# Attention, two dense layers with gates: tokens in five tiles instead of four batches, fills of one PSUM bank

## Chip, cores, metric
The kernel runs on one core of a Trainium2 chip. The metric is the device time of one execution in microseconds (us); smaller is better. TensorE is called PE here, its weight loads PEld, VectorE DVE, ScalarE ACT, GpSimd POOL, and the queue of SyncE, which issues the DMAs, SPq.

## What is computed
Attention over 4 batches of 8 heads, 576 tokens and 64 features per head, in which scores more than tau below the row's maximum are dropped, and then two feed-forward layers over all 2304 tokens:

```python
scores = q @ k.T / 8                                   # (4, 8, 576, 576)
scores = where(scores >= max(scores) - tau, scores, -1e9)
p = exp(scores - max(scores)); p = p / (sum(p) + 1e-9)
x = (p @ v) as 2304 tokens x 512
h = x @ w_in                                           # 512 -> 2048
y = (h * tanh(softplus(h))) @ w_out                    # 2048 -> 512
g = y @ w_gate; z = (silu(g) * (y @ w_val)) @ w_out2   # 512 -> 1536 -> 512
```

All operands are fp32. Each is split into a high part (rounded to fp32r) and a low part (the rest), and a product is three matmuls (high by high, high by low, low by high), or two where one operand holds both parts in its 128 rows.

## The kernel before
**Feed-forward work.** A unit is four 128x128 blocks of weights. There are 68 units per tile of tokens (UNITS): 16 for w_in, 16 for w_out, 24 for the gate and value matrices in turn (gate, value, gate, ...), 12 for the last matrix. A tile is one batch, 576 tokens, and a unit runs it in two halves of 288 columns, each 12 matmuls (4 blocks by 3 products, L455 to L457). A half fills 288 columns of a bank of ps_m, which has three banks in turn: a fill waits until the fill three before it has been read (`emptied`). For w_in, ACT reads the bank with Mish (mish, L652), ACT rounds to g_hi (g_high, L656) and POOL makes g_lo (g_low, L863). For a gate, ACT does tanh (L666) and DVE a product (gate_product, L773), and only then is the bank free; for a value, DVE reads it (s_product, L779), ACT makes g_hi and POOL g_lo (L867).

**Weights.** In tile 0 the 68 units are loaded raw (256 KB, load), rounded on DVE (w_high, L762), their low part made on POOL (w_low, L858), and stored split (512 KB, store, L422); in the other three tiles they are read back split (reload, L431). The ring w_sp has 6 slots, w_raw 3.

**Attention.** A pair of heads has 576 x 2 query rows in 9 chunks of 128: one chunk holds the last 64 rows of each of the two heads, with the products of both heads. For each chunk: scores (8 matmuls of 288 columns, or 4 if the chunk has one head; L481, L482) into a pair of banks, rowmax (L709) on DVE, exp (L628) on ACT, mask and sum (L717) on DVE, thresh and eps on POOL, reciprocal on DVE, norm (L848) on POOL. Then per head 25 transposes (L508, L511) in 6 turns, each one a bank of ps_x, each read by ACT (p_high, L638) and DVE (p_low, L731, L737), and 18 matmuls of 288 columns with v (values, L524 to L526), shifted on ACT (head_shift, L647) and added on DVE (head_add, L747). Per head, q, k and v are loaded into single buffers (load_qkv, L404 to L413) and split: q_high and q_low (L605, L702), k_high and k_low (L611, L824), v_high and v_low (L619, L830). After a batch, x_high (L754, DVE) and x_low (L853, POOL) make the input of its tile.

**Order.** Attention of batch 0 runs alone, with scores in two pairs of banks (ps_s and two banks of ps_m). Attention of batch a+1 is then mixed into the feed-forward units of tile a, with scores in one pair of banks (a chunk waits for the mask of the one before) and three banks of ps_x. The last tile has no attention beside it. The order of all steps on every queue is fixed at build time by `Plan.order`, a list scheduler with a cost, a rank and lags for each step; it picks the step that can start first. A step that needs the exp table is not put inside the 16 Mish units of a tile. Each engine works through its list in that order, with semaphore waits.

Of the kernel before, what the change touches and what calls it, by code (L numbers as in the profile page):

```python
# [11 lines left out]
P = 128  # L12
# [5 lines left out]
KC = 5  # L18
DC, FC1, FC2 = DM // P, F1 // P, F2 // P
UW = 4  # L20
KEY0 = (0, 128, 256, 384, 448)
CHUNKS = 9
P_SLOTS = 10
TURNS = 6
X_USES = TURNS + 2

# [10 lines left out]
W_RING = 6  # L37
W_RAW = 3
LEAD = 5
# [14 lines left out]
def p_slot(pair, ci):  # L54
    return 8 + pair % 2 if ci == 0 else ci - 1


def x_before(k):


    alone = X_USES * HEADS
    if k < alone:
        return k - 4
    return k - 3 if k - 3 >= alone else alone - 4 + k % 3


def unit_steps(u):

    if u in (0, U_G):
        return (0, 0), (1, 0), (0, 1), (1, 1)  # L70
    return (0, 2), (1, 2)


def unit_end(G):
    m, u = divmod(G, UNITS)
    return ("unit", m, u) + unit_steps(u)[-1]


class Plan:
# [12 lines left out]
    def attention(self, a):  # L92
        add = self.add
        alone = a == 0
        near = 0.15 if alone else 0.5
        for h in range(HEADS):
            H = HEADS * a + h
            J, odd = divmod(H, 2)
            q_used = ("scores", CHUNKS * (J - 1) + (8 if odd else 4))
            add("SP", 1.6, 2, ("load_qkv", H), (("q_low", H - 1), 0.1), (("k_low", H - 1), 0.1), (("v_low", H - 1), 0.1))  # L100
            add("ACT", 0.78, 5, ("q_high", H), (("load_qkv", H), 2.4), (q_used, 0.3))
            add("DVE", 0.9, 4, ("q_low", H), (("q_high", H), 0.2))
            add("ACT", 0.68, 5, ("k_high", H), (("load_qkv", H), 2.6), (q_used, 0.3))
            add("POOL", 1.75, 2, ("k_low", H), (("k_high", H), 0.2))
            add("ACT", 0.65, 6, ("v_high", H), (("load_qkv", H), 2.8), (("values", H - 2, 1), 0.3))
            add("POOL", 1.46, 4, ("v_low", H), (("v_high", H), 0.2))
        for j in range(PAIRS):
            J = PAIRS * a + j
            for ci in range(CHUNKS):
                C = CHUNKS * J + ci  # L110
                odd = ci > 4
                back = 2 if alone else 1
                kept = ("tpose", 2 * J - 3, 0) if ci == 0 else ("tpose", 2 * J - 2 + odd, TURNS - 1)
                add("PE", 1.06 if ci == 0 else 0.53, 1, ("scores", C), (("q_low", 2 * J + (ci == 0)), near),
                    (("k_low", 2 * J + (ci == 0)), near), (("mask", C - back), near))
                add("DVE", 0.75, 5, ("rowmax", C), (("scores", C), 0.3))
                add("POOL", 0.12, 0, ("thresh", C), (("rowmax", C), 0.15))
                add("ACT", 0.78, 3, ("exp", C), (("rowmax", C), 0.15), (kept, 0.3), table="exp")
                add("DVE", 0.85, 2, ("mask", C), (("exp", C), 0.2), (("thresh", C), 0.15))
                add("POOL", 0.12, 0, ("eps", C), (("mask", C), 0.15))  # L120
                add("DVE", 0.08, 1, ("recip", C), (("eps", C), 0.15))
                add("POOL", 1.0, 1, ("norm", C), (("recip", C), 0.15))
        for h in range(HEADS):
            H = HEADS * a + h
            J, odd = divmod(H, 2)
            held = ("values", H - (2 if alone else 1), 1)
            for i in range(TURNS):
                ready = ("norm", CHUNKS * J + (0 if i == 0 else 8 if odd else 4))
                add("PE", 0.55, 0, ("tpose", H, i), (ready, near), (self.x_free(H, i), near))
                add("ACT", 0.6 if i else 0.45, 2, ("p_high", H, i), (("tpose", H, i), 0.3), (held, 0.3))  # L130
                add("DVE", 0.68 if i else 0.5, 3, ("p_low", H, i), (("p_high", H, i), 0.2))
            for half in range(2):
                add("PE", 1.32, 0, ("values", H, half), (("p_low", H, TURNS - 1), near), (("v_low", H), near),
                    (self.x_free(H, TURNS + half), near))
                add("ACT", 0.42, 2, ("head_shift", H, half), (("values", H, half), 0.3))
                add("DVE", 0.45, 3, ("head_add", H, half), (("head_shift", H, half), 0.2))
        for j in range(PAIRS):
            y_used = ("unit", a - 1, U_O - 1, 1, 2)
            add("DVE", 0.5, 6, ("x_high", a, j), (("head_add", HEADS * a + 2 * j + 1, 1), 0.15), (y_used, 0.3))
            add("POOL", 1.65, 3, ("x_low", a, j), (("x_high", a, j), 0.2))  # L140

    def x_free(self, H, i):
        H, i = divmod(x_before(X_USES * H + i), X_USES)
        return ("p_low", H, i) if i < TURNS else ("head_add", H, i - TURNS)

    def weights(self, m):
        for u in range(UNITS):
            G = UNITS * m + u
            free = unit_end(G - W_RING)
            if m == 0:  # L150
                self.add("SP", 0.4, 1, ("load", G), (("w_low", G - W_RAW), 0.1), (unit_end(G - LEAD - 3), 0.1))
                self.add("DVE", 0.6, 4, ("w_high", G), (("load", G), 2.8), (free, 0.3), (("store", G - W_RING), 4.0))
                self.add("POOL", 1.47, 2, ("w_low", G), (("w_high", G), 0.2))
                self.add("SP", 0.4, 3, ("store", G), (("w_low", G), 0.1))
            else:
                self.add("SP", 0.4, 0, ("reload", G), (free, 0.1), (("store", G - W_RING), 4.0))

    def moe(self, m):
        add = self.add
        for u in range(UNITS):  # L160
# [7 lines left out]
            elif U_Y <= u < U_G:  # L168
                after.append((("g_low", m, UW * part + UW - 1), 0.3))
            elif u == U_G:  # L170
                after.append((("y_low", m, DC - 2, 1), 0.3))
                late = [(("y_low", m, DC - 1, 1), 0.3)]
            elif u >= U_O:
                after.append((("s_low", m, UW * part + UW - 1), 0.3))
            for half, blocks in unit_steps(u):
                each = late if blocks == 1 else after
                if first and blocks != 1:
                    each = each + [(self.emptied(2 * (FILLS * m + n) + half - 3), 0.3)]
                add("PE", (1.19, 0.4, 1.58)[blocks], 2, ("unit", m, u, half, blocks), *each)
            for half in range(2):  # L180
                done = (("unit", m, u, half, unit_steps(u)[-1][1]), 0.3)
                if u < U_Y:
                    add("ACT", 0.42, 0, ("mish", m, u, half), done, table="mish")
                elif u < U_G:
                    if end:
                        add("ACT", 0.42, 0, ("y_high", m, n - N_Y, half), done)
                        add("DVE", 0.45, 0, ("y_low", m, n - N_Y, half), (("y_high", m, n - N_Y, half), 0.2))
                elif u < U_O:
                    f, value = divmod(n - N_G, 2)
                    if not value:  # L190
                        add("ACT", 0.42, 0, ("gate_tanh", m, f, half), done, table="exp")
                        add("DVE", 0.45, 0, ("gate_product", m, f, half), (("gate_tanh", m, f, half), 0.2))
                    else:
                        add("DVE", 0.45, 0, ("s_product", m, f, half), done, (("gate_product", m, f, half), 0.15))
                elif end:
                    add("DVE", 0.45, 0, ("out", m, n - N_O, half), done)
            if u < U_Y:
                add("ACT", 0.68, 4, ("g_high", m, u), (("mish", m, u, 1), 0.2))
                add("POOL", 1.65, 1, ("g_low", m, u), (("g_high", m, u), 0.2))
            elif U_G <= u < U_O and (n - N_G) % 2:  # L200
                add("ACT", 0.68, 4, ("s_high", m, f), (("s_product", m, f, 1), 0.2))
                add("POOL", 1.55, 1, ("s_low", m, f), (("s_high", m, f), 0.2))
            elif u >= U_O and end:
                add("SP", 0.4, 0, ("keep", m, n - N_O), (("out", m, n - N_O, 1), 0.1))

    def emptied(self, k):
        F, half = divmod(k, 2)
        m, n = divmod(F, FILLS)
        if n < N_Y:
            return "mish", m, n, half  # L210
        if n < N_G:
            return "y_low", m, n - N_Y, half
        if n < N_O:
            f, value = divmod(n - N_G, 2)
            return ("s_product" if value else "gate_product"), m, f, half
# [712 lines left out]
```

## Time and profile before

| | us |
|---|---|
| median of 3 runs | 1235.16 (1234.11 to 1236.33) |
| the profiled execution | 1235.01, of which the span from the first to the last instruction is 1233.2 |
| first matmul starts | 26.55 |
| first feed-forward matmul starts | 168.64 |
| last matmul ends | about 1229.8 |

| engine | busy us | share of the span |
|---|---|---|
| PE | 1150.4 | 93% |
| DVE | 578.4 | 47% |
| POOL | 530.3 | 43% |
| ACT | 476.1 | 39% |

Matmuls are pipelined: a matmul's duration in the trace (about 295 ns for 288 columns) overlaps the next ones. What it costs in a full stream is its pitch, the time from one start to the next.

### The profile page before, as it was taken

The page shows a single profiled execution, that of the slowest core. Times are in us where ns is not written, and L with a number is a line of the kernel's source. Part 1 is how long each engine was busy: PE and PEld are TensorE (multiplying, and loading weights), DVE is VectorE, ACT ScalarE, POOL GpSimd, SP SyncE. Part 2 cuts the span into 40 slices and gives each one's busy share as a digit, 9 for nine tenths or more (in the row PEclk, how much of TensorE's full clock was granted, in tenths as well). Part 3 has the DMA queues.
Part 4 walks back from the last instruction along what each step waited for, and adds up shares of the span by engine and source line. Part 5 has one row for each costly group of instructions (what it writes and reads, how often), then busy time and mean ns, then how long its engine had stood idle before and what let it go on. Part 6 is the DMA issues. An engine that isn't in the chain of part 4 may idle for free.

```text
span 1233.2 us, 21754 instructions
## 1 busy us (share of the span) xinstructions
PE 1150.4 (93%) x8544; PEld 1133.3 (92%) x8544; DVE 578.4 (47%) x1240; ACT 476.1 (39%) x873; POOL 530.3 (43%) x698
## 2 busy tenths in 40 slices
PE   1666689999999999999999998999999999999998
PEld 0656579999999999999999998999999999999998
DVE  2787741366777850255666653045666400002220
ACT  1554544343444344434554435433444204302210
POOL 4455548756677835332444524432443304201210
PEclk9977789999999999999999999999999999999999
DMA  7111127665656554454545455544433465445443
GB/s 243 41 35 44 50 81 256 233 205 195 211 190 218 188 182 171 143 158 135 158 130 162 130 170 154 180 142 140 145 128 120 142 202 174 163 163 171 164 162 107
DMA packets 83765, 190.69 MB, mean 155 GB/s; under 512 B 29904, under 2 KB 29904, under 8 KB 83664
## 3 DMA queue, kind: packets, MB, share of 16 engines
q1 hardware_dynamic: 83664, 189.31, 47.6%
q8 instruction: 68, 1.11, 0.4%
q14 instruction: 33, 0.27, 0.1%
HBM read 148.90 MB, written 40.37 MB: 153 GB/s over the span
## 4 chain that ended last, share of the span: by engine, by line
PE 87%; DVE 5%; POOL 2%; ACT 2%; issue 1%; DMA 1%; SPq 1%; DVEq 0%; ACTq 0%
PE ps_m L455 23%; PE ps_m L457 23%; PE ps_m L456 23%; PE ps_x L511 5%; PE ps_s L481 3%; PE ps_s L482 3%; PE ps_x L524 2%; PE ps_x L525 2%; DVE p_t L717 2%; DMA k_raw<-kt 1%; DVE nmax L709 1%; PE ps_x L508 1%; DVE p_lo_b L737 1%; DVE p_lo L737 1%; PE ps_x L526 1%
## 5 line engine op out<-in xcount | busy, mean ns | idle before, releaser
L455 PE MATMUL ps_m<-x_hi,w_sp 128*128 128x288 f32 x1280 | 380.4, 297 | 5.9 <-ACT g_raw L652 3.3
L457 PE MATMUL ps_m<-x_hi,w_sp 128*128 128x288 f32 x1280 | 378.5, 296 | 0.0
L456 PE MATMUL ps_m<-x_lo,w_sp 128*128 128x288 f32 x1280 | 378.0, 295 | 0.0
L455 PE MATMUL ps_m<-g_hi,w_sp 128*128 128x288 f32 x896 | 265.3, 296 | 0.0
L457 PE MATMUL ps_m<-g_hi,w_sp 128*128 128x288 f32 x896 | 264.2, 295 | 0.0
L456 PE MATMUL ps_m<-g_lo,w_sp 128*128 128x288 f32 x896 | 263.9, 295 | 0.0
L455 PEld LDWEIGHTS ps_m<-x_hi,w_sp 128*128 128x128 f32 x1280 | 241.2, 188 | 7.2 <-ACT g_raw L652 3.8
L456 PEld LDWEIGHTS ps_m<-x_lo,w_sp 128*128 128x128 f32 x1280 | 241.2, 188 | 0.0
L457 PEld LDWEIGHTS ps_m<-x_hi,w_sp 128*128 128x128 f32 x1280 | 241.1, 188 | 0.0
L455 PEld LDWEIGHTS ps_m<-g_hi,w_sp 128*128 128x128 f32 x896 | 168.2, 188 | 0.3
L456 PEld LDWEIGHTS ps_m<-g_lo,w_sp 128*128 128x128 f32 x896 | 168.1, 188 | 0.0
L457 PEld LDWEIGHTS ps_m<-g_hi,w_sp 128*128 128x128 f32 x896 | 168.1, 188 | 0.0
L717 DVE SCALAR_TENSOR_TENSOR p_t<-ps_s,thr,p_t 128x576 f32<-128x576 f32 x126 | 102.7, 815 | 132.3 <-ACT p_t L628 119.2
L628 ACT ACTIVATE p_t<-ps_s,nmax 128x576 f32<-128x576 f32 x126 | 93.2, 740 | 169.5 <-DVE nmax L709 168.5
L863 POOL TENSOR_TENSOR g_lo<-g_raw,g_hi 128x576 fp32r<-128x576 f32 x64 | 91.6, 1432 | 111.3 <-ACT g_hi L656 111.2
L848 POOL TENSOR_SCALAR p_t<-p_t,rcp 128x576 f32<-128x576 f32 x144 | 108.5, 754 | 49.5 <-DVE rcp L724 48.7
L709 DVE TENSOR_REDUCE nmax<-ps_s 128x1 f32<-128x576 f32 x126 | 95.2, 755 | 69.1 <-PE ps_s L482 67.1
L867 POOL TENSOR_TENSOR g_lo<-g_raw,g_hi 128x576 fp32r<-128x576 f32 x48 | 69.9, 1457 | 128.6 <-ACT g_hi L670 128.3
L481 PE MATMUL ps_s<-k_hi,q_sp 128*128 128x288 f32 x280 | 87.4, 327 | 39.2 <-POOL k_lo L824 26.6
L638 ACT ACTIVATE p_hi<-ps_x 128x512 fp32r<-128x512 f32 (+2 forms) x164 | 87.9, 570 | 49.2 <-PE ps_x L511 43.8
L858 POOL TENSOR_TENSOR w_sp<-w_raw,w_sp 128x512 fp32r<-128x512 f32 x68 | 89.2, 1312 | 37.3 <-DVE w_sp L762 37.0
L652 ACT ACTIVATE g_raw<-ps_m 128x288 f32<-128x288 f32 x128 | 51.9, 411 | 133.5 <-PE ps_m L457 133.3
(91 smaller groups left out, 1575.4 us busy)
## 6 DMA issues: line engine op xcount, KB each, us to landing
w_sp<-scratch SPq DMA_DIRECT2D x204, 512.0 KB, 3.3
scratch<-w_sp SPq DMA_DIRECT2D x68, 512.0 KB, 3.0
w_raw<-weights SPq DMA_DIRECT2D x68, 256.0 KB, 3.4
q_raw<-qt SPq DMA_DIRECT2D x64, 144.0 KB, 3.7
k_raw<-kt SPq DMA_DIRECT2D x64, 144.0 KB, 3.7
out_t<-o_sb SPq DMA_DIRECT2D x16, 288.0 KB, 4.1
v_raw<-v SPq DMA_DIRECT2D x32, 128.0 KB, 2.7
v_raw<-v SPq DMA_DIRECT2D x64, 16.0 KB, 2.4
```

Source lines behind the costliest of these rows:

```text
L455: nc.tensor.matmul(ps, w_h, x_h, start=first, stop=False)
L456: nc.tensor.matmul(ps, w_h, x_l, start=False, stop=False)
L457: return nc.tensor.matmul(ps, w_l, x_h, start=False, stop=last)
L481: nc.tensor.matmul(to, q, k_hi[:, e, cols], start=e == heads[0], stop=False)
L628: act.activation(halves(p_t[:, slot, :]), s_banks(C), ACT.Exp, bias=nmax[:, slot:slot + 1]).then_inc(e_ready, 1)
L638: act.activation(to, from_ps, ACT.Copy).then_inc(p_hi_ready, 1)
L709: dve.tensor_reduce(nmax[:, slot:slot + 1], s_banks(C), axis=AX.XY, op=ALU.max, negate=True).then_inc(max_ready, 1)
L717: dve.scalar_tensor_tensor(p, s_banks(C), thr[:, slot:slot + 1], p, ALU.is_ge, ALU.mult, accum_out=sums[:, slot:slot + 1]).then_inc(mask_d ...
L848: pool.tensor_scalar(p_t[:, slot, :], p_t[:, slot, :], rcp[:, slot:slot + 1], 1.0, ALU.mult, ALU.mult).then_inc(norm_done, 1)
L858: pool.tensor_tensor(w_sp[:, slot, 1, :], w_raw[:, u % W_RAW, :], w_sp[:, slot, 0, :].bitcast(F32), ALU.subtract).then_inc(w_ready, 1)
L863: pool.tensor_tensor(g_lo[:, f, :], g_raw[:, f, :], g_hi[:, f, :].bitcast(F32), ALU.subtract).then_inc(g_lo_ready, 1)
L867: pool.tensor_tensor(g_lo[:, f, :], g_raw[:, f, :], g_hi[:, f, :].bitcast(F32), ALU.subtract).then_inc(s_lo_ready, 1)
```

## The change
- **Tiles.** The 2304 tokens are cut into five tiles of 384, 448, 512, 512 and 448, across the batches (TILES). Where a tile has tokens of two batches, attention for it is made in two pieces (PIECES). There are eight pieces, of 384, 192, 256, 320, 192, 384, 128 and 448 queries; each runs all 8 heads, with q of its queries and the whole k and v of its batch. So k and v are loaded and split for 64 heads, before for 32. The 144 chunks stay 144; 16 of them are still shared by two heads, 4 each in the pieces of 192, 320, 192 and 448.
- **Fills.** A unit runs its whole tile in one fill: 12 matmuls of 384 to 512 columns in one bank. ps_m has two banks in turn (M_BANKS), ps_x has two in turn beside feed-forward work (X_BANKS); in attention alone ps_x uses the two banks of ps_m as well. ps_s has four banks: scores use two pairs everywhere.
- **Transposes and values.** A head's 25 transposes are now 5 for each of its chunks (a shared chunk is turned whole for each head), in 5 turns of one block of keys, or 3 turns of two, two and one where they fit. values makes 9 matmuls of the piece's width.
- **Loads.** Two slots each for q, k and v; one DMA for each (the host writes q and k twice, one copy under the other, and lays v out as it lies in the buffer); k and q of a head are issued ahead of v and, for heads 0 to 2, ahead of the first weights. tau is loaded by ACT's queue, and the exp table is loaded at the start.
- **Weights.** Units with even numbers are raw in tile 0 alone and stored there. Units with odd numbers are raw in tiles 0 and 1 and stored in tile 1 (kept_at). So 102 raw loads, 68 stores, 238 reloads. w_high moves from DVE to ACT; w_low is on DVE for every second one and on POOL for the others. w_sp has 7 slots, w_raw 4.
- **The plan.** New costs; within an engine a step of lower rank may be taken if it can start within 0.2 us of the first; chunks of attention are held back so that they spread over 80% of the tile before (PACE).

```diff
-W_RING = 6
-W_RAW = 3
+W_RING = 7
+W_RAW = 4
+X_BANKS, M_BANKS = 2, 2
+TILES = (384, 448, 512, 512, 448)
+PACE = 0.8
+PATIENCE = {"PE": 0.0, "ACT": 0.2, "DVE": 0.2, "POOL": 0.2, "SP": 0.0}
+def kept_at(u):
+    return u % 2
+def low_on_vector(r):
+    return r % 2 == 1
+def turns_of(H):
+    n = queries(H)
+    if n == P:
+        return (0, 1, 2, 3), (4,)
+    if n + n % P <= 2 * P:
+        return (0, 1), (2, 3), (4,)
+    return (0,), (1,), (2,), (3,), (4,)
...
 def moe(self, m):
+        N = TILES[m]
+        mm = 3 * (0.231 if N == 512 else N / 2400 + 0.015)
...
-                back = 2 if C < CHUNKS * PAIRS else 1
-                if C >= back:
-                    pe.wait_ge(mask_done, C - back + 1)
+                if C >= 2:
+                    pe.wait_ge(mask_done, C - 1)
...
-            def load_qkv(H):
-                if H > 0:
-                    sp.wait_ge(q_ready, H)
-                for r in range(2):
-                    sp.dma_start(q_raw[r * DH:(r + 1) * DH, :], qt[H]).then_inc(q_loaded, 16)
...
+            def load_qk(H):
+                if H >= 2:
+                    sp.wait_ge(k_ready, H - 1)
+                sp.dma_start(k_raw[:, slot, :], kt[head]).then_inc(k_loaded[slot], 16)
+                if H >= 2:
+                    sp.wait_ge(q_ready, H - 1)
+                sp.dma_start(q_raw[:, slot, 0:n], qt[head, :, q0:q0 + n]).then_inc(q_loaded[slot], 16)
...
-                if first and blocks != 1:
-                    emptied(2 * (FILLS * m + n) + half - 3)
+                if first and not k0:
+                    emptied(FILLS * m + n - M_BANKS)
...
-                cols = slice(half * HALF, (half + 1) * HALF)
-                for k in (range(UW - 1), range(UW - 1, UW), range(UW))[blocks]:
+                for k in range(k0, k1):
                     w_cols = slice(k * P, (k + 1) * P)
-                    last = product(m_bank(m, n, half), w_sp[:, slot, 0, w_cols], w_sp[:, slot, 1, w_cols],
-                                   r_hi[:, cols], r_lo[:, cols], first and k == 0, end and k == UW - 1)
+                    last = product(m_bank(m, n), w_sp[:, slot, 0, w_cols], w_sp[:, slot, 1, w_cols], *rhs[k],
+                                   first and k == 0, end and k == UW - 1)
```

## Rows read from the trace of the kernel before
**Rows 1.** Page, 40 equal slices: busy tenths of PE, granted clock.
```profile
PE   1666689999999999999999998999999999999998
PEclk9977789999999999999999999999999999999999
```
**Rows 2.** Stretches: us, busy us (instructions) of the engines, granted clock, DMA share, GB/s.
```profile
26.50:168.60 142.10, 93.12 (x512) 83.06 (x512) 104.77 (x229) 71.44 (x125) 71.39 (x130) 0.82 0.17 47
168.60:1229.80 1061.20, 1057.26 (x8032) 1050.24 (x8032) 466.09 (x998) 399.72 (x741) 446.56 (x554) 1.00 0.51 167
...
168.60:300.00 131.40, 131.36 (x977) 130.55 (x978) 59.23 (x125) 53.99 (x100) 89.18 (x97) 0.98 0.63 211
300.00:430.00 130.00, 129.89 (x998) 128.51 (x997) 101.26 (x214) 57.96 (x108) 97.90 (x116) 1.00 0.60 200
```
**Rows 3.** Waits of PE from 168 us to the end: us in total, times, longest.
```profile
PE ps_m L455 <- ACT g_raw L652: 3.3, 1, 3.3
PE ps_m L455 <- POOL x_lo L853: 2.6, 1, 2.6
```
**Rows 4.** Chain that ended last, 0 to 30 us: start, us, what.
```profile
11.46 4.03 POOL w_sp L858 x3
...
16.35 1.11 SPq L404
...
19.03 0.60 SPq L408
...
19.67 4.55 DMA k_raw<-kt
...
24.25 0.69 ACT k_hi L611
...
25.01 1.41 POOL k_lo L824
...
26.55 0.58 PE ps_s L481
```
**Rows 5.** DVE in order of time, last tile: start us, us, operation, idle time before.
```profile
1199.62 0.46 DVE L787 COPY o_sb<-ps_m 128x288 f32<-128x288 f32 x1 [7.48 <-PE ps_m L457]
...
1209.16 0.46 DVE L787 COPY o_sb<-ps_m 128x288 f32<-128x288 f32 x1 [7.48 <-PE ps_m L457]
```
**Rows 6.** PE in order of time around twelve transposes.
```profile
300.34 1.47 PE L511 MATMUL ps_x<-ident,p_t 128*128 128x128 f32 x12
301.57 0.38 PE L481 MATMUL ps_s<-k_hi,q_sp 128*128 128x288 f32 x1
301.79 0.29 PE L482 MATMUL ps_s<-k_lo,q_sp 128*128 128x288 f32 x1
```
**Rows 7.** Groups by line and shape: count, busy us, mean ns, idle before.
```profile
L717 DVE SCALAR_TENSOR_TENSOR p_t<-ps_s,thr,p_t 128x576 f32<-128x576 f32 x126 | 102.7, 815 | 132.3 <-ACT p_t L628 119.2 <-POOL thr L836 12.2
L709 DVE TENSOR_REDUCE nmax<-ps_s 128x1 f32<-128x576 f32 x126 | 95.2, 755 | 69.1 <-PE ps_s L482 67.1
L628 ACT ACTIVATE p_t<-ps_s,nmax 128x576 f32<-128x576 f32 x126 | 93.2, 740 | 169.5 <-DVE nmax L709 168.5
L863 POOL TENSOR_TENSOR g_lo<-g_raw,g_hi 128x576 fp32r<-128x576 f32 x64 | 91.6, 1432 | 111.3 <-ACT g_hi L656 111.2
L858 POOL TENSOR_TENSOR w_sp<-w_raw,w_sp 128x512 fp32r<-128x512 f32 x68 | 89.2, 1312 | 37.3 <-DVE w_sp L762 37.0
...
L737 DVE TENSOR_TENSOR p_lo<-ps_x,p_hi 128x512 fp32r<-128x512 f32 x108 | 70.2, 683 | 22.6 <-ACT p_hi L638 22.4
...
L638 ACT ACTIVATE p_hi<-ps_x 128x512 fp32r<-128x512 f32 x108 | 59.1, 599 | 42.8 <-PE ps_x L511 42.5
...
L652 ACT ACTIVATE g_raw<-ps_m 128x288 f32<-128x288 f32 x128 | 51.9, 411 | 133.5 <-PE ps_m L457 133.3
...
L779 DVE SCALAR_TENSOR_TENSOR g_raw<-g_top,ps_m 128x288 f32<-128x288 f32 x96 | 43.5, 454 | 50.0 <-PE ps_m L457 49.5
```
**Rows 8.** x_high (L754) alone: count, durations in ns min/median/max, first and last start.
```profile
L754 DVE CAST x_hi<-x_raw x16: 450/460/1689, 62.3 to 978.2; 128x576 fp32r<-128x576 f32 x16
```

More of the change, by code:

```diff
@@ L97, in attention @@
             H = HEADS * a + h
[L98 to L103, printed above, removed]
@@ L104, in attention @@
-            add("POOL", 1.75, 2, ("k_low", H), (("k_high", H), 0.2))
-            add("ACT", 0.65, 6, ("v_high", H), (("load_qkv", H), 2.8), (("values", H - 2, 1), 0.3))
-            add("POOL", 1.46, 4, ("v_low", H), (("v_high", H), 0.2))
+            q_used = ("scores", chunks_of(H - 2)[-1]) if H >= 2 else None
+            add("SP", 0.8, 2, ("load_qk", H), (("q_low", H - 2), 0.1), (("k_low", H - 2), 0.1))
+            add("SP", 0.4, 2, ("load_v", H), (("v_low", H - 2), 0.1))
+            add("ACT", 0.2 + 0.00084 * SEQ, 5, ("k_high", H), (("load_qk", H), 2.4), (q_used, 0.3))
@@ L107, in attention @@
+            add("POOL", 1.45, 2, ("k_low", H), (("k_high", H), 0.2))
+            add("ACT", 0.2 + 0.00096 * n, 5, ("q_high", H), (("load_qk", H), 2.6), (q_used, 0.3))
+            add("DVE", 0.2 + 0.0012 * n, 4, ("q_low", H), (("q_high", H), 0.2))
+            add("ACT", 0.46, 6, ("v_high", H), (("load_v", H), 2.5), (("values", H - 2), 0.3))
+            add("POOL", 0.88, 4, ("v_low", H), (("v_high", H), 0.2))
         for j in range(PAIRS):
             J = PAIRS * a + j
[L109 to L122, printed above, removed]
@@ new lines, in attention @@
+            for C in range(FIRST[J], FIRST[J + 1]):
+                _, e, i = CHUNK[C]
+                H = 2 * J + (1 if e < 0 else e)
+                kept = ("tpose", last_reader(C - P_SLOTS), len(turns_of(last_reader(C - P_SLOTS))) - 1) if C >= P_SLOTS else None
+                pace = None
+                if not alone:
+                    first = FIRST[PAIRS * (LAST_OF[tile - 1] + 1)]
+                    last = FIRST[PAIRS * (LAST_OF[tile] + 1)]
+                    pace = unit_end(UNITS * (tile - 1) + int(PACE * UNITS * (C - first) / (last - first)))
+                add("PE", 1.06 if e < 0 else 0.53, 1, ("scores", C), (("q_low", H), near), (("k_low", H), near),
+                    (("mask", C - 2), near), (pace, 0.0))
+                add("DVE", 0.76, 5, ("rowmax", C), (("scores", C), 0.3))
+                add("POOL", 0.28, 0, ("thresh", C), (("rowmax", C), 0.1))
+                add("ACT", 0.74, 3, ("exp", C), (("rowmax", C), 0.1), (kept, 0.3), table="exp")
+                add("DVE", 0.9, 2, ("mask", C), (("exp", C), 0.15), (("thresh", C), 0.1))
+                add("POOL", 0.2, 0, ("eps", C), (("mask", C), 0.1))
+                add("DVE", 0.1, 1, ("recip", C), (("eps", C), 0.1))
+                add("POOL", 0.76, 1, ("norm", C), (("recip", C), 0.1))
@@ L123, in attention @@
         for h in range(HEADS):
             H = HEADS * a + h
[L125 to L140, printed above, removed]
@@ new lines, in attention @@
+            add("PE", 9 * max(0.1, n / 2400 + 0.015), 0, ("values", H), (("p_low", H, len(turns) - 1), near), (("v_low", H), near),
+                (self.x_free(USE0[H] + len(turns)), near))
+            add("ACT", 0.17 + 0.00084 * n, 2, ("head_shift", H), (("values", H), 0.3))
+            add("DVE", 0.17 + 0.00101 * n, 3, ("head_add", H), (("head_shift", H), 0.2), (("x_low", tile - 1, h // 2), 0.1))
+        if a == LAST_OF[tile]:
+            width = TILES[tile]
+            for j in range(PAIRS):
+                y_used = unit_end(UNITS * (tile - 1) + U_O - 1) if tile else None
+                add("DVE", 0.1 + 0.001 * width, 6, ("x_high", tile, j), (("head_add", HEADS * a + 2 * j + 1), 0.15), (y_used, 0.3))
+                add("POOL", 0.1 + 0.00236 * width, 3, ("x_low", tile, j), (("x_high", tile, j), 0.2))
@@ L180, in moe @@
[L180 to L196, printed above, removed]
@@ L197, in moe @@
-            if u < U_Y:
[L198 to L204, printed above, removed]
@@ L886, in _ @@
                     x_low(*args)
-                elif step == "w_low":
+                elif step == "w_low" and not low_on_vector(RAW_AT[args[0]]):
                     w_low(*args)
```

689 lines of the change are left out of this document (378 added, 311 removed).

## Prediction
> **What bounds the kernel now.** I read the slices of the page first, then the stretches, PE's waits, the chain that ended last, and single rows for prices. The slices split the run in two [rows 1]: up to 168.6 us PE is idle or six tenths busy at a reduced clock, and from there it is full. From 168.6 to 1229.8 PE is busy 1057.3 of 1061.2 us [rows 2], and only two of its waits count there, 3.3 and 2.6 us [rows 3]. So there are two regimes. In the first, 168.6 us long, the work of batch 0 is a chain through DVE, ACT and POOL: from 26.5 us on DVE is busy 104.8 of 142.1 us, 74%, more than any other [rows 2]. In the second, the time is PE's number of matmuls times their pitch. After the last matmul 3.4 us remain. The sum is made against the span, 1233.2; the execution took 1235.0, 1.8 more, and the median of the runs is 1235.2, so 1.8 is added at the end.
>
> **Start: 26.5 becomes about 8.5.** The chain shows who sets the first matmul [rows 4]: POOL does three w_low (11.5 to 15.5), the weights' queue entries follow, then q and k of head 1 are issued at 16.4 and 19.0, k lands at 24.2, ACT and POOL split it (0.7 + 1.4), and PE starts. Head 1 is needed at once because the first chunk is shared by two heads, and its load waits since there is one buffer. After the change head 0's k is first in the queue, head 1 has its own slot, and the piece of 384 has no shared chunk. Sum: issue at 1, landing 4.6 later, 0.7 + 1.4, waits between: 7.7; some transfers now meet, so I take 8.5 (bounds 7.7 and 11).
>
> **Attention alone: 142.1 becomes about 100.5.** 24 chunks instead of 36. A 128-row chunk costs DVE 0.755 + 0.815 + 0.16 for its reciprocal = 1.73 [rows 7]. DVE's other prices follow from two rows: 288 columns 0.454 and 512 columns 0.683 give 0.16 us plus 1.02 ns a column [rows 7], 0.55 for 384. So before: 36 x 1.73 = 62; turns 8 heads x 4.07 = 33; adds 16 x 0.454 = 7; q_low and x_high about 7: 109. After: 24 x 1.73 = 41.5; turns 8 x 5 x 0.55 = 22; adds 8 x 0.55 = 4.4; q_low, x_high and three w_low, which DVE gets, about 8.5: 76.5. Ratio 0.70; with the idle share kept, 142.1 x 0.707 = 100.5. Bounds: all of DVE's idle time stays (76.5 + 37.3 = 113.8), or a third of it goes with the shorter pairs (90). First feed-forward matmul: 8.5 + 100.5 = 109 instead of 168.6: **-59.6** (bounds -70 and -44). Nothing hides this: PE can do nothing before it.
>
> **Feed-forward matmuls.** Between two reads of finished sums lie 72 matmuls: 1209.16 - 1199.62 = 9.54, a pitch of 132.5 ns for 288 columns [rows 5]. At 2.4 GHz the columns are 120.0 of it, 12.5 come on top. Before: 68 x 12 x 2 x 4 = 6528 matmuls, 865.0 us. After: 68 x 12 x 5 = 4080, the same 2304 x 816 columns, 783.4 us of columns. If 12.5 ns stays per matmul: 783.4 + 51.0 = 834.4. If the extra grows with the columns (20 ns for 461): 865.0. No row shows more than 288 columns, and at 12 transposes of 128 columns the pitch is 0.103 [rows 6], so the extra is no constant below 288; I take the middle, 849.7: **-15.3** (bounds -30.6 and 0). The planner's new costs, 15 to 18 ns extra, say the same. The Trainium skill ("TensorE: Matmul & The Clock Gate", Wait — 56ns, not 53.3ns?) gives back-to-back matmuls N/2.4 ns plus about 2.5 ns; that would be 122.5 at 288 columns, and this trace has 132.5, so the row decides; by the page the sum after would be 793.6.
>
> **Attention that moves beside the feed-forward work.** Before, 24 heads were there; each costs PE 5 units of scores (a unit: 4 matmuls, 0.53) = 2.65, transposes 25 x 0.10 + 3 switches x 0.09 (the matmul after a run of transposes starts 0.22 later instead of 0.13 [rows 6]) = 2.77, values 18 x 0.1325 = 2.39: 7.8, 187 in all. Check: 865 + 187 = 1052 of the 1061.2 measured [rows 2]; 9 are left for the waits and the slow first matmuls. After, all but the first piece is there: scores 120 chunks, 16 of them double, 136 x 0.53 = 72; transposes 136 chunk readings x 5 = 680 x 0.10 = 68, and about 130 switches x 0.09 = 12, since two banks allow runs of two turns; values 72 matmuls for each of seven pieces at 0.118, 0.128, 0.148, 0.118, 0.176, 0.109 and 0.203 (192, 256, 320, 192, 384, 128, 448 columns, between the pitches of 128 and 288 columns and 16 ns over the columns above) = 72. Together 224: **+37** (bounds +32 and +43). That is the price of the shorter first part; the last tile, which nobody accompanies, is shorter too, which is why all of it fits in four tiles.
>
> **New waits beside the feed-forward work: +8** (bounds 0 and +30). Today a fill has two fills, 3.18 us, to be read. With two banks it has one: 12 x 0.176 = 2.1 us for the tile of 384, 2.4 for 448, 2.8 for 512. The longest reading is a gate's, tanh on ACT and product on DVE: 0.49 + 0.55 and some 0.15 of handing over, 1.2 in the first tile, if both engines are free. If an exp (0.74) and a mask (0.82) have just begun, 2.8, and PE waits 0.65; in the tiles of 448 and 512 that worst case costs about 0.5 and 0.25. Twelve gates in four tiles: 20 at the very most from this. Today's worst, 2.5 against 3.18, costs nothing, as the trace shows. I take a third, 6.5, and 1.5 for one more table load in PE's way as the 3.3 [rows 3]. The higher bound takes in the load of the engines, which I count for the first tile, some 197 us long (143 of units and 54 of attention): ACT gets 68 w_high x 0.60 = 41, k_high and v_high of 16 heads 18, in all about 149; POOL 34 w_low x 1.31 = 45, 28 of 384 columns at 0.98 = 27, k_low and v_low 37, chunks 35, in all about 149; DVE about 131. That is 76%, 76% and 66%. Between 300 and 430 us today POOL is at 75% and DVE at 78% with PE unbroken [rows 2], so this is no bound by itself. DMA: 68 raw loads, 34 stores and 16 heads, 45 MB in 197 us, 228 GB/s; the second tile 54 MB in 224 us, 241. Today 211 GB/s take 63% of the DMA engines [rows 2], so 72% at most: hidden, by units asked for seven fills ahead. The doubled loads and splits of k and v cost PE nothing under this cover; without it 32 more k_low of 1.43 would be 46 us of POOL.
> What is edited without a term: scores in a second pair of banks beside the feed-forward work (nobody waits for the first today), the end (a drain of 448 columns is 0.16 us longer, its transfer shorter).
>
> **Sum.** 1233.2 - 59.6 - 15.3 + 37 + 8 = 1203.3; with 1.8, **1205**.
>
> **Rivals.**
> *The two terms at their good ends* (22%): first part 8 us shorter still, extra of 12.5 ns: 1205 - 8 - 13 = 1184. For it: pairs of 6 chunks in 10 slots of p need not wait for the pair before; against: no row of long matmuls.
> *The pitch gives nothing and PE waits* (14%): extra in proportion (+15) and waits of 15 instead of 8: 1227. For it: no long matmul in the trace.
> *Slower* (7%): readings of single banks decide. Between two fills one gate's tanh and product, queued behind attention, exceed the fill. 272 fills stand beside attention; from 0.15 us each (41 us, against 8 assumed: 1238) it ends on the other side. Against: exp is kept out of the Mish units, and DVE and ACT are a third and a quarter idle.
> *w_low on DVE* (4%): x_high, which reads and writes SBUF alone, takes 0.46 as a rule and up to 1.69 [rows 8], as if held up by POOL's work. If 51 w_low on DVE behave like this and DVE's queue is late by 1.2 us each, and half of that reaches PE: +30, 1235. The Trainium skill ("SBUF — State Buffer", Who interferes with whom) has DVE and GpSimd share a port pair as an exclusive lock; the row agrees in that one operation is stretched by 1.2 us.
> *Not what it says* (3%): with fills of 512 columns the extra vanishes: 783 of columns alone would give 1139; rows at 288 speak against it.
> My own case has 50%.
>
> **Range and chances.** The likeliest gives 1205; its own range is 1192 to 1218. To hold 8 in 10, the range takes in the good ends and most of the bad pitch: 1180 to 1228. 0.2%, 2.5 us, is about what a measurement of this kernel can tell from no change. Slower by more than that, over 1237.6: most of the third rival and a part of the fourth, 0.07; within it 0.03; faster 0.90.
>
> **What would show it.** First score matmul near 8.5 and first feed-forward matmul near 109; reads of finished sums in the last tile (448) 36 matmuls apart: 7.3 us (7.2 if the extra is constant, 7.4 if in proportion); PE's idle time after the first feed-forward matmul under 15 us, its releasers L666 and gate_product's successors; DMA under 75% in the first two tiles. The prediction is wrong if attention alone is not scaled by its chunks, if a 512-column matmul's pitch is off 229 ns by more than 6, or if PE's waits beside attention add up to more than 20 us.

## The result
The changed kernel takes 1174.9 us (median; 1173.4 to 1177.7), the one before 1235.7 beside it: ratio 0.951, 95% interval 0.949 to 0.953. The prediction said 1205 with a range of 1180 to 1228: the direction was right, the gain was twice as large as forecast (61 us, not 30), and the time lies below the range. The profiled execution took 1177.7 us with a span of 1175.9.

The page of the changed kernel, in slices, beside [rows 1]:

```profile
PE   4667999999999999999999999999999999999998
...
PEclk9886999999999999999999999999999999999999
```

PE is at four tenths in the first slice, where it was at one, and it is full from the fifth slice on, where before this was the seventh. The stretches, in the columns of [rows 2]:

```profile
8.00:108.00 100.00, 64.23 (x300) 56.51 (x301) 75.03 (x160) 57.37 (x106) 60.96 (x99) 0.82 0.36 112
108.00:1173.00 1065.00, 1064.19 (x5798) 963.86 (x5796) 520.39 (x1022) 510.17 (x951) 532.73 (x671) 1.00 0.64 206
```

In the second one PE is idle 0.8 us of 1065, with two banks, 22% more DMA traffic than before (232 MB against 191, whole run) and ACT busy 510 us instead of 400. All waits of PE from 90 us on, which answer to [rows 3]:

```profile
PE ps_m L564 <- POOL x_lo L947: 3.4, 1, 3.4
PE ps_m L617 <- POOL p_t L941: 2.6, 1, 2.6
PE ps_m L628 <- issue: 1.2, 1, 1.2
PE ps_s L588 <- DVE q_sp L807: 0.4, 1, 0.4
PE ps_x L617 <- DVE x_raw L847: 0.2, 1, 0.2
```

The first three belong to attention alone and its end. No wait for the reading of a feed-forward bank (L745, L870) is left: the term of 8 us for new waits measured 0.6 at most.

The first matmul starts at 7.9, on q of head 0, where [rows 4] ended at 26.55:

```profile
7.90 0.58 PE L588 MATMUL ps_s<-k_hi,q_sp 128*128 128x288 f32 x1 [7.90 <-DVE q_sp L807]
```

Reads of finished sums in the last tile (448 columns), which answer to [rows 5]:

```profile
1150.98 0.62 DVE L882 COPY o_sb<-ps_m 128x448 f32<-128x448 f32 x1 [6.67 <-PE ps_m L566]
1158.28 0.62 DVE L882 COPY o_sb<-ps_m 128x448 f32<-128x448 f32 x1 [6.67 <-PE ps_m L566]
```

36 matmuls in 7.30 us: 202.8 ns, which is 186.7 for the columns and 16 more, the middle that the sum took. In unbroken streams of the whole trace I found a pitch of 176 ns for 384 columns, 203.5 for 448 and 228 for 512 (the prediction had 229 for the last).

From both traces I added up, over PE's full stretch, the gap from each matmul's start to the next one's, by the kind of the matmul that begins it. A gap also holds a wait, if there is one, so the columns sum to the stretch:

| kind | before, 168.6 to 1229.8 | after, 104.3 to 1172.8 | change | predicted |
|---|---|---|---|---|
| feed-forward | 877.0 | 860.6 | -16.4 | -15.3 |
| scores | 66.3 | 76.1 | +9.8 | +8 |
| transposes | 59.2 (600) | 61.9 (680) | +2.7 | +14 |
| values | 58.6 | 69.9 | +11.3 | +15 |
| new waits | | in the rows above | 0 | +8 |
| PE's full stretch | 1061.2 | 1068.5 | +7.3 | +30 |
| until the first feed-forward matmul | 168.6 | 104.3 | -64.3 | -59.6 |

With the end, 0.3 us shorter, this is the whole difference of the spans, 57.3 us.

One thing makes the rows differ from the terms of the prediction. The matmul behind a run of transposes holds the next one up for longer than usual. The prediction counted this with the transposes; in the table it stands in the row of the matmul that follows. Over all runs of transposes it adds up to 6.7 us before (74 runs, 3.9 us of it in the feed-forward row) and to 13.3 us after (154 runs, 9.6 us in the feed-forward row). Moved to the transposes, they change by +9.3 us instead of +2.7, and the feed-forward row by -22.1 instead of -16.4.

### The profile page after: what moved, and what is told of

The parts are those of the page before. It is cut to its first block, busy times and chain, and to the rows that moved or that the text cites. A ratio compares the mean times of both kernels' runs of the same rounds, so it can differ in the third digit from the quotient of the medians.

```text
span 1175.9 us, 17588 instructions
## 1 busy us (share of the span) xinstructions
PE 1128.5 (96%) x6096; PEld 1020.5 (87%) x6096; DVE 597.6 (51%) x1187; ACT 571.3 (49%) x1062; POOL 596.0 (51%) x777
## 4 chain that ended last, share of the span: by engine, by line
PE 90%; POOL 4%; DVE 3%; issue 1%; ACT 1%; DMA 0%; SPq 0%; ACTq 0%; DVEq 0%
PE ps_m L564 23%; PE ps_m L566 23%; PE ps_m L565 23%; PE ps_x L617 7%; PE ps_s L588 3%; PE ps_s L589 3%; PE ps_x L629 3%; PE ps_x L628 3%; POOL p_t L941 1%; PE ps_m L617 1%; POOL k_lo L919 1%; DVE p_t L820 1%; PE ps_x L630 1%; DVE q_sp L807 1%; DVE nmax L813 1%
## 5 line engine op out<-in xcount | busy, mean ns | idle before, releaser
L564 PE MATMUL ps_m<-x_hi,w_sp 128*128 128x512 f32 (+2 forms) x800 | 301.9, 377 | 3.5 <-POOL x_lo L947 3.4
L566 PE MATMUL ps_m<-x_hi,w_sp 128*128 128x512 f32 (+2 forms) x800 | 296.5, 371 | 0.0
L565 PE MATMUL ps_m<-x_lo,w_sp 128*128 128x512 f32 (+2 forms) x800 | 296.1, 370 | 0.0
L564 PE MATMUL ps_m<-g_hi,w_sp 128*128 128x448 f32 (+2 forms) x560 | 211.5, 378 | 0.0
L565 PE MATMUL ps_m<-g_lo,w_sp 128*128 128x448 f32 (+2 forms) x560 | 207.1, 370 | 0.0
L566 PE MATMUL ps_m<-g_hi,w_sp 128*128 128x448 f32 (+2 forms) x560 | 207.1, 370 | 0.0
L564 PEld LDWEIGHTS ps_m<-x_hi,w_sp 128*128 128x128 f32 x800 | 150.8, 189 | 20.0 <-issue 4.0
L566 PEld LDWEIGHTS ps_m<-x_hi,w_sp 128*128 128x128 f32 x800 | 150.8, 188 | 18.1
L565 PEld LDWEIGHTS ps_m<-x_lo,w_sp 128*128 128x128 f32 x800 | 151.0, 189 | 15.3
L958 POOL TENSOR_TENSOR g_lo<-g_raw,g_hi 128x448 fp32r<-128x448 f32 (+2 forms) x80 | 96.2, 1204 | 97.9 <-ACT g_hi L749 97.5
L732 ACT ACTIVATE p_hi<-ps_x 128x384 fp32r<-128x384 f32 (+8 forms) x220 | 101.9, 478 | 66.9 <-PE ps_x L617 62.4
L745 ACT ACTIVATE g_raw<-ps_m 128x448 f32<-128x448 f32 (+2 forms) x80 | 44.5, 556 | 162.8 <-PE ps_m L566 162.8
L963 POOL TENSOR_TENSOR g_lo<-g_raw,g_hi 128x448 fp32r<-128x448 f32 (+2 forms) x60 | 71.6, 1193 | 99.6 <-ACT g_hi L761 98.3
L617 PE MATMUL ps_x<-ident,p_t 128*128 128x128 f32 x740 | 112.4, 280 | 8.0 <-POOL p_t L941 6.5
L566 PEld LDWEIGHTS ps_m<-g_hi,w_sp 128*128 128x128 f32 x560 | 105.1, 188 | 12.7
L564 PEld LDWEIGHTS ps_m<-g_hi,w_sp 128*128 128x128 f32 x560 | 105.2, 188 | 10.6
```

Source lines behind the costliest of these rows:

```text
L564: nc.tensor.matmul(ps, w_h, x_h, start=first, stop=False)
L565: nc.tensor.matmul(ps, w_h, x_l, start=False, stop=False)
L566: return nc.tensor.matmul(ps, w_l, x_h, start=False, stop=last)
L617: last = nc.tensor.transpose(to[:, c, at:at + P], keys, ident)
L732: act.activation(to, from_ps, ACT.Copy).then_inc(p_hi_ready, 1)
L958: pool.tensor_tensor(g_lo[:, f, cols], g_raw[:, f, cols], g_hi[:, f, cols].bitcast(F32), ALU.subtract).then_inc(g_lo_ready, 1)
```

## Experiments
All are edits of the changed kernel (one of the kernel before) and are given as ratios to the kernel before, beside 0.951 for the change itself. "First" is the start of the first feed-forward matmul, "full stretch" from there to the last read of a sum; the changed kernel has 104.3 and 1068.5.

**The size of the first tile, up.**

```diff
-TILES = (384, 448, 512, 512, 448)
+TILES = (512, 448, 448, 448, 448)
```

> The changed kernel with tiles of 512, 448, 448, 448, 448. Theory A (price of attention alone is DVE's chain per chunk): 32 chunks alone, first feed-forward matmul near 134 us (+30), attention beside feed-forward work 8 us cheaper for PE, feed-forward matmuls the same: about 1197 us. Rival (the first part is set by latencies per pair of heads, not by chunks): first feed-forward matmul near 110, about 1173 us.

1196.7 us, ratio 0.969 (0.967 to 0.971). The total is theory A's to within 1 us, but two of its parts are off and cancel: the first feed-forward matmul comes at 126.9, 7 us earlier than worked out, and the full stretch is 1065.4, 5 us longer. From 384 to 512 queries alone costs 22.6 us, 2.8 us for each of the 8 added chunks; the rival, latencies per pair of heads, would have left it near 110. Neither price is met: theory A's 30 us are 3.7 a chunk.

**The size of the first tile, down.**

```diff
-TILES = (384, 448, 512, 512, 448)
+TILES = (256, 512, 512, 512, 512)
```

> The changed kernel with tiles of 256, 512, 512, 512, 512. Theory A (the time is DVE's chain alone and then PE's matmuls times their pitch, waits do not matter): attention alone goes from 24 to 16 chunks, first feed-forward matmul near 79 us instead of 104.3 (-25); attention beside it costs PE 16 us more (144 score units instead of 136, 720 transposes instead of 680, values 77.5 instead of 69.4), feed-forward matmuls +1: about 1167 us, 8 under the changed kernel. Theory B (the other engines bound a tile that is too short for the attention beside it): tile 0 is then about 156 us of PE work, and counted from rows ACT, POOL and DVE each get 152 to 153 us in it (68 w_high, 34 + 34 w_low, 32 chunks, 16 heads of k and v), so PE waits 15 to 35 us there: 1182 to 1202 us.

1214.2 us, ratio 0.983 (0.981 to 0.985): slower than either theory said. The first feed-forward matmul does come early, at 75.7, and the full stretch is 1134.4 instead of 1068.5. Its stretches and its largest waits of PE:

```profile
140.00:200.00 60.00, 56.59 (x445) 54.18 (x444) 54.57 (x108) 44.28 (x96) 52.33 (x64) 1.00 0.81 273
200.00:260.00 60.00, 48.11 (x332) 45.73 (x332) 47.15 (x104) 36.99 (x74) 42.66 (x62) 0.89 0.64 212
260.00:350.00 90.00, 79.28 (x359) 64.48 (x359) 24.33 (x50) 42.44 (x80) 45.11 (x46) 0.86 0.49 158
...
PE ps_x L628 <- DVE p_hi L836: 13.3, 9, 3.1
```

The sums of tile 0 are all read at 227.4 us, and the input of the next tile is ready much later (this view gives the durations and then the first and last start, 260.9 and 292.0):

```profile
L947 POOL TENSOR_TENSOR x_lo<-x_raw,x_hi x4: 1255/1262/1268, 260.9 to 292.0; 128x512 fp32r<-128x512 f32 x4
```

The same view of the changed kernel, whose last matmul of tile 0 starts at 301.4:

```profile
L947 POOL TENSOR_TENSOR x_lo<-x_raw,x_hi x4: 1145/1231/1595, 275.9 to 288.1; 128x448 fp32r<-128x448 f32 x4
```

For 65 us PE has attention and nine matmuls of the next tile, now with two banks for the turns, and at a reduced clock (0.73 on average from 230 to 300 us). The place named by theory B was right. Its reason, full engines, was not: DVE's share is 76% from 78 to 260 us and POOL's 78%. What the traces show is that attention for the next tile is ready at nearly the same time in both kernels, 293.3 and 289.7 us, although the units beside it end 76 us apart. From the first feed-forward matmul on, that is 218 us for 512 queries and 185 for 448. It takes a time of its own, and pacing does not make it (off, it is 195, see below); which part of its chain sets it no run separates.

**In between.**

```diff
-TILES = (384, 448, 512, 512, 448)
+TILES = (320, 448, 512, 512, 512)
```

> The changed kernel with tiles of 320, 448, 512, 512, 512. A first tile of 256 lost because its units were over at 228 us while the attention beside it (512 queries) lasted to 293. Here units of tile 0 take 120 us instead of 143.6 beside the same attention of 448 queries. Theory A (attention of 448 queries needs about 190 us beside units, PE has 176 us of work): first feed-forward matmul near 92 (-12), PE work +8, waits and slow clock +15: 1180 to 1190. Theory B (448 queries keep up): 1171.

1197.2 us, ratio 0.968 (0.967 to 0.970). Worse than both theories, but the full stretch grows by 21 us, close to theory A's 23. In tile 0 PE is idle again:

```profile
101.00:288.00 187.00, 177.00 (x1242) 172.41 (x1243) 136.54 (x258) 130.55 (x264) 149.88 (x178) 0.98 0.73 241
```

Attention for tile 1, 448 queries as in the changed kernel, is ready at 293.6 us, 6 us after the last matmul of tile 0. Theory A fails in attention alone: the first feed-forward matmul comes at 100.8, only 3.5 us earlier and not 12, though a pair has five chunks instead of six. Why attention alone gains so little I did not settle; a width of 320 brings back the chunk that two heads share, and with it the wait for head 1.

**Short matmuls.**

```diff
-                for k in range(k0, k1):
+                if first and end and (k0, k1) == (0, 2):
+                    return
+                split = first and end and k0 == 2
+                for half in range(2 if split else 1):
+                    cols = slice(half * width // 2, (half + 1) * width // 2) if split else slice(0, width)
+                    for k in range(0 if split else k0, k1):
...
```

> The changed kernel, but in 38 of the 68 units of a tile the 12 matmuls are made as 24 of half the columns (192, 224 or 256), into the same bank: 2280 more matmuls, the same columns. Theory A (a floor near 110 ns for short matmuls, from weight loading, with pitches of 0.1095, 0.115 and 0.120): +53 us, 1228. Theory B (a constant extra of 15.8 ns per matmul): +36 us, 1211. Theory C (extra in proportion to the columns): no change, 1175.

1232.9 us, ratio 0.998 (0.997 to 0.999): 58 us more, theory A's floor and not the constant. In this edit all matmuls of a split unit stand behind the point where it was cut in two, so attention's place between them moves a little too. The stream of 192-column matmuls:

```profile
110.56 0.27 PE L565 MATMUL ps_m<-x_lo,w_sp 128*128 128x192 f32 x1
110.67 0.28 PE L566 MATMUL ps_m<-x_hi,w_sp 128*128 128x192 f32 x1
110.78 0.27 PE L564 MATMUL ps_m<-x_hi,w_sp 128*128 128x192 f32 x1
```

They start 0.11 apart where the columns take 0.080; averaged over their gaps, 192 and 224 columns both cost 0.112, 256 cost 0.121. What sets the floor, the loading of weights or something else, no run separates. The edit gives back all but 2 us of what the change won. It does not mean that long matmuls were the gain: 288 columns lie above this floor, and by the pitches the change from 288 to 461 was worth 17 us.

**A longer reading of the bank.**

```diff
+                act.activation(dump[:, 0:TILES[m]], m_bank(m, N_G + 2 * f), ACT.Tanh, scale=0.5).then_inc(dumped, 1)
                 act.activation(g_top[:, f, 0:TILES[m]], m_bank(m, N_G + 2 * f), ACT.Tanh, scale=0.5).then_inc(tanh_ready, 1)
```

> The changed kernel with each gate's tanh made twice on ACT (the first into a spare buffer), which lengthens the reading of a gate's bank by 0.5 to 0.6 us, 60 times. Theory A (a bank's reading has slack within one fill of 2.1 to 2.8 us even with two banks): 0 to +5 us. Theory B (two banks are at the edge, as the prediction's term of 8 us assumed): each gate beside attention costs 0.2 us or more, +10 to +30 us.

1179.0 us, ratio 0.954 (0.952 to 0.956), an interval that overlaps that of the change; the profiled spans are 1176.2 and 1175.9, and the full stretch is 1069.4. The medians are 4 us apart, but the executions of this run, at granted clocks of 0.983 to 0.985, took 1176.8 to 1180.0 us, and that of the changed kernel at 0.984 took 1177.7; its other three had 0.990 or 0.991. Nearly all of the half microsecond more for each of 60 gates is absorbed: two banks have slack (theory A).

**Scores in one pair of banks beside feed-forward work.**

```diff
-                    (("mask", C - 2), near), (pace, 0.0))
+                    (("mask", C - (2 if alone else 1)), near), (pace, 0.0))
...
-                if C >= 2:
-                    pe.wait_ge(mask_done, C - 1)
+                back = 2 if C < FIRST[ALONE_HEADS // 2] else 1
+                if C >= 2:
+                    pe.wait_ge(mask_done, C - back + 1)
```

> The changed kernel with scores in one pair of banks beside feed-forward work: a chunk's scores wait for the mask of the chunk before, a chain of 0.76 + 0.74 + 0.82 us and handing over, 2.6 us. Theory A (PE has units of 2.1 to 2.8 us to put between two chunks, as in the kernel before): 0 to +3 us. Theory B (attention beside the first, short tile does not keep up without the second pair, as with a first tile of 256): +10 us or more, with PE waits before tile 1.

1194.7 us, ratio 0.967 (0.965 to 0.968): theory B. PE's largest wait is then at the starts of tiles, three times and 9.9 us in all, where the changed kernel waits for this once, 3.4 us:

```profile
PE ps_m L564 <- POOL x_lo L948: 9.9, 3, 3.4
```

The full stretch is 1086.3, +18. Attention for tile 1 is ready at 307.3 us, the last matmul of tile 0 starts at 290.6; attention for tile 2 is ready at 543.0, the last matmul of tile 1 starts at 532.6.

**All low parts of the weights on POOL.**

```diff
 def low_on_vector(r):
-    return r % 2 == 1
+    return False
```

> The changed kernel with all 102 w_low on POOL. In tile 0 POOL then has 149 + 34 x 1.35 = 195 us of work for some 197 us of PE work. Theory A (POOL becomes the bound there): +10 to +25 us, with PE waits before 300 us. Theory B (the split does not matter, only PE's matmuls do): within 2 us of the changed kernel.

1218.9 us, ratio 0.986 (0.984 to 0.987): 44 us more, beyond theory A's bound. The stretches of this kernel, and then the same of the changed one:

```profile
200.00:250.00 50.00, 48.87 (x285) 48.58 (x284) 11.99 (x22) 24.56 (x48) 46.75 (x41) 1.00 0.89 293
250.00:300.00 50.00, 43.48 (x278) 40.47 (x277) 38.94 (x83) 32.00 (x65) 34.80 (x52) 0.93 0.61 193
300.00:400.00 100.00, 84.73 (x399) 74.11 (x400) 30.73 (x64) 48.72 (x92) 55.15 (x63) 0.83 0.47 152
```

```profile
200.00:250.00 50.00, 49.98 (x330) 48.99 (x328) 44.90 (x93) 39.44 (x79) 44.60 (x58) 1.00 0.75 240
250.00:300.00 50.00, 50.00 (x321) 49.59 (x320) 32.55 (x56) 28.04 (x55) 33.00 (x33) 1.00 0.71 232
300.00:400.00 100.00, 100.00 (x565) 93.85 (x564) 52.62 (x111) 60.20 (x111) 62.69 (x85) 1.00 0.75 250
```

POOL is 93% busy between 200 and 250 us, DVE 24%: I read this as attention standing behind the weights in POOL's list. The bill comes from 250 to 400 us: PE is idle 22 us of 150 and clocked down, as with the tile of 256. The last matmul of tile 0 starts at 276.3, and attention for tile 1 is ready at 343.4.

**All units raw in tile 0.**

```diff
 def kept_at(u):
-    return u % 2
+    return 0
```

> The changed kernel with all 68 units raw and stored in tile 0 and read back from tile 1 on. Tile 0 then moves 63 MB in about 197 us of PE work, 318 GB/s against 228, and rows of the kernel before put a full set of DMA engines at about 335 GB/s (211 at 63%). Theory A (that is too near the limit, PE waits for weights in tile 0): +10 to +30 us. Theory B (transfers stay hidden behind a ring of seven, and tile 1 is relieved of 34 roundings): within 2 us of the changed kernel.

1178.9 us, ratio 0.954 (0.952 to 0.956), full stretch 1069.4. The median is 4 us above the change, outside theory B's 2 us and far below theory A's 10; the interval overlaps that of the change, and no transfer holds up PE, as theory B has it. Between 140 and 180 us this kernel has the first line, the changed one the second:

```profile
140.00:180.00 40.00, 39.62 (x262) 38.78 (x261) 32.73 (x64) 30.63 (x58) 33.13 (x44) 1.00 0.93 328
```

```profile
140.00:180.00 40.00, 39.65 (x264) 39.12 (x263) 31.57 (x63) 30.45 (x58) 32.67 (x43) 1.00 0.70 228
```

DMA engines 93% busy with 328 GB/s cost PE nothing that shows here. Storing over two tiles is worth at most the few us by which the medians differ, and the spans (1175.8 and 1175.9) do not show those.

**Pacing off.**

```diff
-PACE = 0.8
+PACE = 0.0
```

> The changed kernel with the plan's pacing off (PACE 0): attention beside a tile starts as early as it can instead of spreading over 80% of it. Theory A (an unbroken PE needs the engines' work spread): +5 to +15 us, as chunks crowd the first units of each tile. Theory B (order hardly matters as long as PE has something to do): within 3 us.

1186.8 us, ratio 0.961 (0.959 to 0.963): +12, theory A. The full stretch is 1081.4, while the first feed-forward matmul starts 4 us earlier. Here attention for tile 1 is ready in time (295.0 us; the last matmul of tile 0 starts at 307.9). The loss is inside tile 0, which takes 11 us longer. This kernel, then the changed one:

```profile
104.00:308.00 204.00, 195.97 (x1235) 191.96 (x1234) 140.27 (x259) 136.23 (x266) 151.89 (x180) 0.98 0.67 217
```

```profile
104.00:301.50 197.50, 196.63 (x1248) 194.22 (x1249) 135.63 (x259) 136.98 (x266) 154.96 (x181) 0.99 0.70 228
```

**Weights ahead of k and q.**

```diff
-                raw_free = ("w_low", RAW[r - W_RAW]) if r >= W_RAW else ("load_v", 2)
+                raw_free = ("w_low", RAW[r - W_RAW]) if r >= W_RAW else None
```

> The changed kernel, but the first four loads of weights are issued ahead of k and q of head 0. Theory A (each us of start is a us of the run): k of head 0 is issued 1.9 us later and its transfer shares the DMA engines with 1 MB of weights, first score matmul near 12 instead of 7.9, +4 us, 1179. Theory B (attention alone takes the delay up, because later heads are loaded anyway): 0 to +1 us.

1175.7 us, ratio 0.952 (0.950 to 0.953). The first score matmul starts at 10.95, three us later, and the first feed-forward matmul at 102.8, 1.5 earlier: theory B, this delay is absorbed.

**The kernel before with q and k first.**

```diff
-(("w_low", G - W_RAW), 0.1)
+(("w_low", G - W_RAW) if G >= W_RAW else ("load_qkv", 1), 0.1)
```

> The kernel before, with one edit to its plan: its first weights are loaded after q, k and v of heads 0 and 1. Its single buffers stay. Theory A: POOL's three w_low and the queue entries of the weights go from ahead of head 1, first score matmul near 17.5 instead of 26.5, -9 us, 1226. Rival (the single buffers and DMA time, not the weights, set the start): first score matmul after 23, -3 us or less.

1227.4 us, ratio 0.994 (0.992 to 0.995). The first matmul starts at 16.35 instead of 26.55, the first feed-forward matmul at 159.6 instead of 168.6: theory A, though 7 us and not its 9, since the full stretch grows by 2.5. So 7 us of the 61 are to be had in the old kernel by this alone.

**Transposes twice.**

```diff
+                        nc.tensor.transpose(to[:, c, at:at + P], keys, ident)
                         last = nc.tensor.transpose(to[:, c, at:at + P], keys, ident)
```

> The changed kernel with every transpose issued twice (800 more, 680 of them beside feed-forward work). In the trace of the changed kernel the gaps that begin with a transpose add up to 61.9 us for 680, 0.091 each, where the prediction took 0.10 each and 0.09 more for each of 130 changes to other work, 80 us. Theory A (within a run a transpose costs 0.107, and the last one of a run is followed early, which pays for the slower start behind it): 680 x 0.107 = +73 us beside feed-forward work. Theory B (0.091 is what a transpose costs): +62. If attention alone grows too, its share is read off at the first feed-forward matmul.

1254.0 us (two runs), ratio 1.014 (1.012 to 1.016). The full stretch is 1139.4, 70.8 more for 680: 0.104 for each, nearer to theory A than to B. The first feed-forward matmul starts 6 us later.

## Why the prediction was wrong
The span was forecast as 1203.3 us and measured 1175.9, 27 us less. The largest part is a term that did not occur (new waits, 8 us); 7 us are in the price of attention beside the feed-forward work, 5 in waits and slow first matmuls that were carried over, 5 in the time until the first feed-forward matmul, 2 in the pitch.

**Regimes: right.** Both kernels are a chain of attention alone and then a full PE; the table above closes to the span.

**Start: right.** 7.9 against 8.5. The kernel before gains 7 us from this part alone, as the chain in [rows 4] said. Once the start is near 8 us, though, 3 more do not matter.

**Attention alone: near, 4 us too long.** 96.4 us from the first matmul to the first feed-forward matmul against 100.5 (the sum used a ratio of 0.707 where its own counts give 0.70, which is 1 us). As a rule, DVE's work is rougher than this one hit suggests. The step from 256 to 384 queries costs 3.6 us a chunk, that from 384 to 512 costs 2.8, and 320 queries take 91.7 us from the first matmul, where a line between 256 and 384 gives 82.5.

**Feed-forward matmuls: right, but the row hides it.** By the pitches 816 matmuls in each of five tiles take 848 us (176, 203.5, 228, 228 and 203.5 ns), against 865.0 before: -17, where -15.3 was said. The constant of 12.5 of the 288-column row would have given -31. That the row of the table shows -16.4 is partly luck: 6 us more of slower starts behind transposes are in it, and 5 us less of waits and slow first matmuls. The rule of the Trainium skill ("TensorE: Matmul & The Clock Gate", Wait — 56ns, not 53.3ns?) would give, as an estimate, 189 ns at 448 columns; the trace has 203.

**New waits: the first step that failed, 0 instead of +8.** I reckoned that an exp and a mask just begun would now and then hold up a gate's reading. No wait of PE for such a reading is left in the trace, and the run with each tanh made twice shows slack for half a microsecond more. So the 8 us priced a danger that this order does not run into.

**Attention beside feed-forward work: the second step that failed, +30 instead of +37.** That is 9.0 for the scores, 9.3 for the transposes with the slower starts behind them, and 11.3 for the values. The mechanism, more work for PE, was right; two prices were too high. For the transposes I took 0.10 each and 0.09 for each of 130 changes to other work. The changed kernel's trace shows what a change is:

```profile
501.15 0.60 PE L617 MATMUL ps_x<-ident,p_t 128*128 128x128 f32 x4
501.50 0.45 PE L564 MATMUL ps_m<-g_hi,w_sp 128*128 128x448 f32 x1
501.79 0.37 PE L565 MATMUL ps_m<-g_lo,w_sp 128*128 128x448 f32 x1
502.00 0.36 PE L566 MATMUL ps_m<-g_hi,w_sp 128*128 128x448 f32 x1
```

Four transposes take 0.35 to the next start, and the gap behind is 0.29 instead of 0.21: 0.43 in all, 0.11 for each. In [rows 6] twelve take 1.23 and 0.09: again 0.11 each. It holds for the 146 runs of two to eight transposes in this trace, whose medians all lie at 0.110 for each (the 8 single ones cost 0.117). Over all 154 runs the last transposes are followed 12.5 us early and the matmuls behind them 13.3 us late. So the slower start behind a run is paid for by an early end of the run; it is no price of its own, and more and shorter runs cost nothing. By that price the term would have been 75 instead of 80, and before 66: +9 instead of +14. Almost 4 us more lie in the values (11.3 instead of 15): 192 and 256 columns cost 0.112 and 0.119 in the trace, and I had taken 0.118 and 0.128.

**What was carried over.** The 9 us of waits and slow first matmuls in the kernel before were left in the sum. In its feed-forward row 8 us are left beside pitch and slower starts, 3.3 of them one wait ([rows 3]); in the changed kernel 3 are left. I have not taken that apart further.

**What had no term.** The danger of the rival "slower" is real in another place. It is not single readings against one fill; it is attention that must be finished when the tile beside it is. In the changed kernel it is, with 12 us to spare in tile 0. Two edits that I priced at nothing carry this: without the second pair of banks for scores +20 us by the medians, without the split of w_low +44. The third, pacing (+12 without it), does something else: attention is in time without it too, but PE then waits 8 us inside tile 0 instead of 1. Each was measured by undoing it alone.

**Work of the other engines: right in number, wrong in reading.** The count for tile 0 (POOL 76%, DVE 66%) was near the rows (from 104 to 300 us POOL 78%, DVE 69%, ACT 70%; from 150 to 250 us POOL 88% and DVE 89%), and no bound. I concluded that the cover was ample. With all of w_low on POOL, 87% of tile 0, it is gone, and what is lost is paid after the tile at a granted clock of 0.73 (276 to 344 us). DMA: right, 70% and 73% in the first two tiles, and without harm even at 93%.

**The rivals.** That of w_low on DVE saw its row come: w_low on DVE takes 0.90 on average and q_low of 384 columns 1.01, more than 0.16 us plus 1.02 ns a column. But it reached PE nowhere, and the split is the largest single support of the result. "The two terms at their good ends" came nearest by its number, 1184, and not by its reasons: the extra of 12.5 ns did not come, and the first part was 5 us shorter, not 8. Its 13 us for the pitch should have been 15 by the sum's own bound.

**The range.** It reached to 1180, for the case that two terms ended well. All terms but the scores ended on the same side, and the median lies 2.8 us below the profiled execution. The sum of the bounds that I had written down, with waits of 0, would have held 1175.

## What to carry over
Where two kinds of work share a full engine, the small one has to be over when the big one is: compare the time that its own chain needs with the length of its partner, tile by tile, before a first tile is made shorter. When gaps are added up by kind of work, say in which row a delay stands that one kind causes and the next one pays, or a match with a term can be an accident. Price a change of work on PE over the whole run of short matmuls and the gap behind, not as an addition to their mean. When several uncertain terms are costs that may not occur at all, let the range reach to all of them at zero.

## What the runs showed of the hardware
Matmuls of 128, 192 and 224 columns all cost 0.112 us in unbroken streams; 256 cost 0.119 to 0.121, 288 0.1325, 384 0.176, 448 0.203, 512 0.228. So the price is flat up to 224 columns, and my line from 128 to 288 columns was too high in between. A transpose of 128 columns costs 0.110 with the slower start behind its run, and 0.104 when 680 are added to runs that exist. With 328 GB/s of DMA traffic at 93% of the engines, behind a ring of seven slots, no wait of PE for a transfer shows in the trace.
